# Reordering one unit of an attention stage on TensorE and VectorE

## What is computed

```python
B, H, S, D = 4, 8, 768, 48
mag = np.sqrt(a_re * a_re + a_im * a_im)
scale = np.minimum(mag, 0.999) / (mag + 1e-06)
a_re_n, a_im_n = (a_re * scale, a_im * scale)
for t in range(S):
    ar, ai = (a_re_n[:, :, t, :, None], a_im_n[:, :, t, :, None])
    new_re = ar * S_re - ai * S_im
    new_im = ar * S_im + ai * S_re
    kv = np.einsum('bhd,bhe->bhde', k[:, :, t], v[:, :, t])
    S_re, S_im = (new_re + kv, new_im)
    y[:, :, t] = np.einsum('bhd,bhde->bhe', q[:, :, t], S_re)
x = y in rows of (batch, time), 384 wide
x = dense mixture of 8 experts (384 -> 1024 -> 384) with gates from softmax and 8 rounds of normalising
x = mixture where each row goes to one expert
```

## Time and profile before

| | |
|---|---|
| profiled execution | 2640.12 us, span 2638.4 us |
| TensorE busy | 2457.6 us, 93% |
| VectorE busy | 1156.7 us, 44% |
| ScalarE busy | 748.2 us, 28% |
| attention stage | up to about 627 us: the last copy of y starts at 627.2 |
| TensorE clock | mean 0.96 of full; 7 to 9 tenths in the slices of the attention, 9 in the dense stage |

### The profile page before, as it was taken

One profiled execution on the slowest core, in us unless ns is written; L12 is line 12 of the kernel. 1 busy time (PEld: TensorE's weight loads), 2 busy tenths in 40 slices (PEclk: granted clock), 3 DMA queues, 4 the chain that ended last, 5 costly groups with the idle time before them and its releaser, 6 DMA issues. The chain is left out here.

```text
span 2638.4 us, 41452 instructions
## 1 busy us (share of the span) xinstructions
PE 2457.6 (93%) x14250; PEld 2296.0 (87%) x14251; DVE 1156.7 (44%) x2533; ACT 748.2 (28%) x1293; POOL 188.4 (7%) x176
## 2 busy tenths in 40 slices
PE   0499999999999999999999999999999999589998
PEld 0376676778999999999999999999999999488897
DVE  6776767543443333333333333333333332475433
ACT  4455555333111111111121121112111112254322
POOL 0000000001011011011010010010010100022221
PEclk9997888889999999999999999999999999699999
DMA  3011111111000000000000000000000011343210
GB/s 121 28 37 66 49 67 49 34 34 49 1 25 12 12 25 2 22 24 0 24 24 0 24 24 0 24 24 0 24 24 0 24 43 37 102 146 133 78 39 21
DMA packets 44717, 96.81 MB, mean 37 GB/s; under 512 B 4101, under 2 KB 26651, under 8 KB 44640
## 3 DMA queue, kind: packets, MB, share of 16 engines
q1 hardware_dynamic: 40672, 84.97, 9.5%
q0 software_dynamic: 3968, 10.82, 1.3%
HBM read 161.83 MB, written 10.81 MB: 65 GB/s over the span
## 5 line engine op out<-in xcount | busy, mean ns | idle before, releaser
L991 PE MATMUL bank<-x_parts,w_hi 128*128 (+1 forms) x3072 | 783.3, 335 | 0.1
L876 ACT ACTIVATE h_hi<-bank 128x384 fp32r<-128x384 f32 x512 | 250.2, 492 | 1250.1 <-PE bank L991 1250.0
L991 PEld LDWEIGHTS bank<-x_parts,w_hi 128*128 128x128 f32 x3072 | 554.3, 188 | 0.2 <-DVEq L913 0.2
L945 DVE SCALAR_TENSOR_TENSOR h_lo<-bank,h_hi 128x384 fp32r<-128x384 f32 x512 | 284.2, 557 | 576.9 <-ACT h_hi L876 576.9
L991 PE MATMUL bank<-x_parts,w_lo 128*128 (+1 forms) x1536 | 513.8, 335 | 0.0
L1003 PE MATMUL bank<-w_hi,h_hi 128*128 128x384 f32 x1536 | 513.3, 334 | 0.0
L1003 PE MATMUL bank<-w_hi,h_lo 128*128 128x384 f32 x1536 | 513.1, 334 | 0.0
L1003 PE MATMUL bank<-w_lo,h_hi 128*128 128x384 f32 x1536 | 513.0, 334 | 0.0
L965 DVE SCALAR_TENSOR_TENSOR mixed<-bank,gate,mixed 128x384 f32 (+1 forms) x336 | 207.7, 618 | 442.4 <-PE bank L1003 442.4
L991 PEld LDWEIGHTS bank<-x_parts,w_lo 128*128 128x128 f32 x1536 | 288.9, 188 | 0.0
L1003 PEld LDWEIGHTS bank<-w_hi,h_lo 128*128 128x128 f32 x1536 | 288.4, 188 | 0.0
(11 more groups left out here) (199 smaller groups left out, 2218.7 us busy)
## 6 DMA issues: line engine op xcount, KB each, us to landing
routed_w_raw<-in_moe_w SPq DMA_DIRECT2D x64, 1536.0 KB, 6.8
w_raw<-in_moe_w SPq DMA_DIRECT2D x32, 768.0 KB, 6.0
q_k<-in_qk SPq DMA_DIRECT2D x24, 512.0 KB, 3.7
decay<-in_a SPq DMA_DIRECT2D x20, 528.0 KB, 4.8
v_rows<-in_v SPq DMA_DIRECT2D x24, 192.0 KB, 2.4
mixed_rows<-mixed SPq DMA_DIRECT2D x4, 1152.0 KB, 4.6
decay<-in_a SPq DMA_DIRECT2D x4, 432.0 KB, 4.9
routed_x<-mixed_rows,gather_now POOLq DMA_INDIRECT x31, 3.1
```

The source lines that it names most:

```text
L876: nc.scalar.activation(h_parts[par][0][:, c, :], h_bank[c], ACT.Relu).then_inc(h_hi, 1)
L945: nc.vector.scalar_tensor_tensor(out=h_parts[par][1][:, c, :], in0=h_bank[c], scalar=0.0, in1=h_parts[par][0][:, c, :].bitcast(F32), op0=A ...
L991: last = nc.tensor.matmul(h_bank[c].rearrange("p (u s) -> p u s", u=SUB), w1_parts[half][w][:, k, c * PT:(c + 1) * PT], mem.x[:, bass.ds(b ...
```

## The change

VectorE's list for a unit: the two steps of `invert` and `divide` move behind later steps of the scan; `add_squares_of_a` moves forward, ahead of the third `sums`; the second `scale` follows the first at once, ahead of `decay_state`. ScalarE's list: the copy of the imaginary k moves behind `guess_inverse`. TensorE's list: even scores, real k transposes, odd scores, sum of squares, imaginary k transposes, logits, all state products (real, then imaginary), x, y. The identity product behind the keys (`keep_warm(kt_re)`) is gone. The four identity products behind y stay for units 0 to 17 and are gone for units 18 to 23.

```diff
                 product(p, 2)
-                invert(a, 0)
-                sums(p, 2)
-                invert(a, 1)
-                product(p, 3)
                 if p + 1 < UNITS:
                     add_squares_of_a(p + 1)
+                sums(p, 2)
+                product(p, 3)
                 sums(p, 3)
+                invert(a, 0)
+                product(p, 4)
+                invert(a, 1)
+                sums(p, 4)
                 divide(a)
-                product(p, 4)
+                product(p, 5)
                 add_state(u)
-                sums(p, 4)
+                sums(p, 5)
                 scale(a, LEFT)
-                product(p, 5)
+                scale(a, RIGHT)
+                product(p, 6)
                 decay_state(u, RE)
-                sums(p, 5)
+                sums(p, 6)
                 decay_state(u, IM)
-                product(p, 6)
-                scale(a, RIGHT)
-                sums(p, 6)
                 new_state(u)
...
+                def place_k_rows(part, bank):
+                    act.wait_ge(k_back, 2 * kept(u) + part + 1)
+                    if u:
+                        act.wait_ge(y_done, u)
+                    nc.scalar.activation(krow[:, part, :, :], pairs(bank), ACT.Copy).then_inc(k_rows, 1)
+
                 if passes_on(u):
-                    for part, bank in enumerate((kt_re, kt_im)):
-                        act.wait_ge(k_back, 2 * kept(u) + part + 1)
-                        if u:
-                            act.wait_ge(y_done, u)
-                        nc.scalar.activation(krow[:, part, :, :], pairs(bank), ACT.Copy).then_inc(k_rows, 1)
+                    place_k_rows(RE, kt_re)
                 if u + 1 < UNITS:
                     guess_inverse(u + 1)
+                if passes_on(u):
+                    place_k_rows(IM, kt_im)
...
+                def turn_k(part, bank):
+                    if kept(u):
+                        pe.wait_ge(k_rows, 2 * kept(u) - 1 + part)
+                    for pair in range(PAIRS):
+                        last = nc.tensor.transpose(pairs(bank)[:, pair, :], qk[:, par, K, part, pair, :], ident[:, :])
+                    last.then_inc(k_back, 1)
+
                 pe.wait_ge(scaled, 2 * u + 2)
-                if passes_on(u):
-                    for part, bank in enumerate((kt_re, kt_im)):
...
                 if u:
                     pe.wait_ge(masked, 2 * u)
                 for h in range(0, H, 2):
                     last = score(h)
                 last.then_inc(scored, 1)
+                if passes_on(u):
+                    turn_k(RE, kt_re)
+                for h in range(1, H, 2):
+                    last = score(h)
+                last.then_inc(scored, 1)
                 if u + 1 < UNITS:
                     sum_squares(u + 1)
+                if passes_on(u):
+                    turn_k(IM, kt_im)
                 if u >= 2:
                     pe.wait_ge(y_copied, u)
                     logits(u - 2)
                 pe.wait_ge(v_landed[u % 3], 16 * (u // 3 + 1))
                 if passes_on(u):
-                    pe.wait_ge(k_rows, 2 * kept(u) + 1)
                     if kept(u):
                         pe.wait_ge(state_read, kept(u))
-                for h in range(1, H, 2):
-                    if passes_on(u):
-                        add_to_state(RE, h - 1)
-                    last = score(h)
-                last.then_inc(scored, 1)
-                if passes_on(u):
-                    pe.wait_ge(k_rows, 2 * kept(u) + 2)
-                    for pair in range(PAIRS):
-                        add_to_state(RE, 2 * pair + 1)
-                        for h in (2 * pair, 2 * pair + 1):
-                            last = add_to_state(IM, h)
+                    for part in (RE, IM):
+                        pe.wait_ge(k_rows, 2 * kept(u) + 1 + part)
+                        for h in range(H):
+                            last = add_to_state(part, h)
                     last.then_inc(kv_done, 1)
                 if u:
                     turn_x(u - 1)
-                if passes_on(u):
-                    keep_warm(kt_re)
...
-                if u + 1 < UNITS:
+                if u + NCH < UNITS:
                     for n in range(4):
                         keep_warm(sc_a)
```

More of the change, by code:

```diff
@@ L645, in add_to_state @@
                                             start=True, stop=True)
-                pe.wait_ge(scaled, 2 * u + 2)
-                if passes_on(u):
-                    for part, bank in enumerate((kt_re, kt_im)):
-                        if kept(u):
-                            pe.wait_ge(k_rows, 2 * kept(u) - 1 + part)
-                        for pair in range(PAIRS):
-                            last = nc.tensor.transpose(pairs(bank)[:, pair, :], qk[:, par, K, part, pair, :], ident[:, :])
-                        last.then_inc(k_back, 1)
+                def turn_k(part, bank):
[4 more added lines that the diff above has]
+                    last.then_inc(k_back, 1)
+                pe.wait_ge(scaled, 2 * u + 2)
                 if u:
```

## The result

The changed kernel takes 2571.17 us (median of four, 2571.01 to 2572.75), against 2640.75 for the kernel before: a ratio of 0.9743, 95% interval 0.9726 to 0.9760. The forecast was 2573. The profiled execution took 2571.04 us, with a span of 2569.3.

What follows compares the result with a forecast made beforehand. It took loops 1 to 16 as closed by a 21.2 us chain through squares, logits, odd scores and second mask, TensorE partly slow. Terms -40, -2, -5, -21 sum to -68: 2640.1 to 2573 us; eight in ten 2550 to 2620.

Steps and rivals of the forecast that it cites:

- main loops: Attention stage, the twelve of loops 1 to 16 other than 5, 6, 11, 12: 20.5 us each forecast, from 22.3.
- S: Moment VectorE ends a unit's second scaling; a loop runs from one to the next, named by the unit whose scores it computes.
- the chain: Loops 1 to 16: state, squares, sum of squares, squares of a, addition, next S; 19.45 us at full clock.
- Loops 5 and 11: Last chunk of a batch, no keys or state: 21.5 us forecast including 1.5 for the clock, against 24.2.
- Loops 6 and 12: Loops where the previous unit's y waits for no state, so squares end early: 17.1 us forecast against 23.7.
- rival A: Most attention units: slow clock outlives the sum of squares, through products and y; 2600 us, chance 0.17.
- The way to unit 18: From S of unit 17 to unit 18's first score: 20.5 us forecast against 25.7, so -5.
- Units 18 to 22: Last units, no scan left, TensorE sheds identity products: 79 us forecast against 99.7, so -21.
- rival C: Short of ten wide records a unit, the clock stays low for most of a unit; slower, 2664 us, chance 0.08.
- a wait grow: Loops 1 to 16: TensorE idles from S + 4.65 to S + 7.0 in front of the sum of squares.
- B: Later squares and the new wait give back all but 5 us of loops 1 to 16's gain; 2617 us, chance 0.10.
- D: Second mask never closed the loop, squares set it then as now; no change, 2640 us, chance 0.05.

Runs made afterwards that it cites:

- third experiment: Changed kernel with two identity products in front of the sum of squares in units 0 to 17; 2559.90 us, ratio 0.9673.
- first experiment: Changed kernel with VectorE's list as it was before, TensorE's and ScalarE's lists new; 2548.98 us, ratio 0.9640.
- sixth experiment: Kernel before with only the four identity products behind y removed in units 18 to 23; 2647.18 us, ratio 1.0007.
- last experiment: The 2523.67 us kernel with the identity product behind the state products put back; 2516.12 us, ratio 0.9531.
- 2523.67 us kernel: Changed kernel with VectorE's old list, ScalarE's squares before the y copy, extra identity products in each batch's last and first units; 2523.67 us, ratio 0.9532.
- the filling products: Extra identity products in units 5, 11, 17 and each batch's first unit; removed from the 2523.67 us kernel: 2536.63 us, ratio 0.9589.

## Why the prediction was right, step by step

**The main loops.** Forecast 20.5, measured (325.8 - 22.0 - 21.1 - 20.3 - 16.5) / 12 = 20.5. The marks of loop 14, as offsets from S: state 2.15 forecast, 2.10 measured; squares 6.95 and 6.93; idle time of TensorE 2.35 and 2.31; wait of VectorE 1.4 plus 1.5 where the clock falls, 2.69; addition to the next S 7.33 and 7.24. That the chain closes the loop, and not VectorE's 18.1 or TensorE's load, is shown by four runs that change one thing each: cutting the chain at the copy of y (17.8), shortening it by the old VectorE list (17.5), and adding TensorE work that costs nothing (2570.92) or pays (2559.90).

**Four terms were off and cancelled.** That the mean came out at 20.5 to the tenth is luck. The loop at full clock is 18.9 to 19.3 (third experiment), not 19.45: less .3. The clock was low in the sum of squares of every main loop, not of two in three: the sum took 2.9 to 3.8 us in all twelve, where 1.98 is its time at full clock: plus .45. And loop 16 was counted with the other eleven, but the decays scanned there are those of unit 23, the last, so that there are no squares of a of a later unit to add or to wait for; it took 17.4 us, which is .3 off the mean. The other eleven took (245.9 - 17.4) / 11 = 20.8. And the fall was not always at the forecast place. In nine of the twelve it came with the idle time of 2.2 to 2.3 us in front of the squares. In loops 1, 7 and 13 TensorE did not wait for the squares: it idled 1.8 or 2.2 us in front of the scores, and the clock fell before they were through. These three took 21.5, 21.3 and 21.6 us, which puts .2 on the mean. Loop 7:

```profile
251.99 2.29 PE L643 MATMUL bank<-scaled_q_k 64*128 64x128 f32 x16 [1.77 <-DVE scaled_q_k L333]
254.22 1.11 PE L655 MATMUL bank<-ident,scaled_q_k 128*128 128x128 f32 x4
...
259.00 3.78 PE L628 MATMUL bank<-squares,ident 128*128 128x512 f32 x4
```

**Loops 5 and 11**: 21.5 forecast, 22.0 and 21.1 measured. **Loops 6 and 12**: 17.1 forecast, 20.3 and 16.5 measured. Loop 6 is where rival A came true: unit 5 ran at half clock for 17 us, its y included (6.7 us), and TensorE began unit 6's scores at 235.5, 3.9 behind S. Unit 11 had one short fall, and loop 12 was .6 under the forecast.

**The way to unit 18**: -5 forecast, -7.8 measured, since y of unit 17 was not slow. **Units 18 to 22**: 79 forecast, 76.6 measured (12.5, 19.2, 14.1, 14.6, 16.2 us). Unit 18 was forecast at 12.7; unit 19 had the half clock of rival C for 13.4 us.

**What the prediction did not see** is not in its total but in its parts. It wrote that the VectorE move makes "a wait grow" and adds one, and did not draw the conclusion that the move costs more than it gives: by its own numbers, as the first experiment's expectation adds them up, the old list with the new TensorE order would have been 17.5 or 17.8. Measured, the TensorE and ScalarE order alone gives 0.9593; the whole change gives back a third of that. It also counted the identity product removed behind the keys among what was to "make the room"; in the changed kernel putting either kind back costs nothing that the ratios tell, so that most of the room must come from the idle time that the chain leaves.

**The rivals.** B (nothing left in loops 1 to 16) is out by 37 us there, D (masks never closed the loop) by the waits. C is real in places: in the sixth experiment removing wide products from the kernel before gained nothing, at a clock of 0.77. The clock did fall in all twelve loops, as the rule of the Trainium skill on transposes ("TensorE: Matmul & The Clock Gate", Part 4: PE-mode transpose) would have had it; but loops 1 to 16 of the last experiment have the same transposes between the same scores at a clock of 1.00. What differs is TensorE's idle time, 1.7 us in all there (276.7 - 275.0) for 36.6 in the changed kernel (325.8 - 289.25); whether transposes count for less is not told by these runs.

## What to carry to other kernels

When a wait is removed, walk the new loop with the old durations and look for the chain that closes it; then ask of each moved instruction which side of that chain it lies on. A change in several parts can be right in its sum and carry a part that costs a third of it, so each engine's list is worth a run of its own. An idle time of two microseconds in front of a wide product can cost another 1.5 by the clock, and work put into it for nothing can pay.

## What the runs showed of the hardware

TensorE's granted clock went to 1.2 GHz in nine main loops of the changed kernel behind idle times of 2.2 to 2.3 us that followed 64-row scores, and in the three others, and in four units of the 2523.67 us kernel, during the scores, behind idle times of 0.7 to 2.4 us in front of them. The length of the idle time alone does not decide: in the first experiment 0.98 us in front of the sum of squares left it at 1.98 us in unit 1, and 0.99 went with 3.25 in unit 3. In several orders the clock stayed low for 17 to 24 us, through scores, narrow state products and y; it came back in wide identity products and sums of squares. In the kernel before, 20 such products less in the last units left the stretch at 102.9 us for 99.7, with the clock at 0.77 for 0.90. Executions of one kernel spread from 2527 to 2546 us without the filling products, and from 2522 to 2525 with them. The mean clock of the former runs from 0.978 to 0.970, but the executions of 2537 and 2546 us both have 0.970, so that the clock is not shown to make the whole of the spread.
